# Attention stage of a fused attention and two-FFN kernel: order of one score product, one PSUM bank, SyncE's queue and VectorE's low parts

## The chip, the cores and the metric

The kernel runs on one core of a Trainium2 chip. The metric is the device time of one execution in microseconds (us). The core has TensorE (PE in the profile; its weight loads are PEld), VectorE (DVE), ScalarE (ACT), GpSimd (POOL) and SyncE (SP), which here only issues DMAs. Each engine runs its own instruction list in order and waits on semaphores.

## The reference, cut to what matters

```python
scores = scale * np.matmul(q, k.transpose(0, 1, 3, 2))      # B, H, S, D = 4, 8, 576, 64
scores = np.where(causal, -1e9, scores); scores -= scores.max(-1, keepdims=True)
a = np.exp(scores); a /= a.sum(-1, keepdims=True) + 1e-09
local = np.matmul(a, v)
q_p = phi(q)                                                # elu(q) + 1
mem_out = (q_p @ M_prev) / ((q_p @ z_prev)[..., None] + 1e-6)
attn = g * mem_out + (1 - g) * local                        # g = sigmoid(beta) per head
x = _moe_ref(attn as [2304, 512], ...)                      # silu(x @ w_gate) * (x @ w_val) @ w_out
return _moe2_ref(x, ...)                                    # g(x @ w_in) @ w_out
```

## The kernel before, in words

The 32 heads are worked off as 16 pairs. The 576 rows of a head are one block of 64 rows and four blocks ("tiles") of 128. A pair has four steps, tile 4 first (576 columns wide), then 3, 2 and 1 (448, 320, 192), and the two 64-row blocks of its heads together form one small product, F (`scores_f`, L1413 to L1419), that writes 64 columns of PSUM bank 1. Scores of tile 4 lie in banks 0 and 1 for the first head and in banks 2 and 3 for the second; tile 3 lies in bank 0 (first head) and bank 1 (second head); tiles 2 and 1 in banks 2 and 3.

TensorE's list is a software pipeline of rounds (L1530 to L1557). Round p holds: the scores of tile 4 of pair p; the "turns" of pair p-1 (transposes of the exponentiated rows, `turn`, in nine groups in the order of `TURNS`, each group in the PSUM bank that `BANK` names, group (1, 0) with one more transpose of the reciprocal sums); F of pair p; the last turn group (1, 1); the scores of tiles 3, 2 and 1 of pair p; and the products with the values of pair p-1 (`values`). F and tile 3 wait until VectorE has taken the maxima of both heads of tile 4 (semaphore `maxed`, one count per head). A turn group waits until the last content of its bank is copied away (`copied_under`).

VectorE's round p (L1161 to L1197): the reciprocal of the sums of pair p-1 (`sums_inverse`), the two outputs of pair p-2 (`out_x`, which need the broadcast sums `rbc`), the copy of turn group (4, 1), the maxima of tile 4, the copy of group (2, 1), `norm_q` and the maxima of tile 3, then `rnorm_q` (whose first instruction is L1064), the maxima of tiles 2 and 1 and of F, small scales (`mem_scale`), `phi` of the next pair, in rounds 5, 6, 8 and 9 a low part of a weight (`up_low`, L1131) and in rounds 10 to 16 a low part of the first FFN's input (`x_low`, L1140), and last `mem_scale(j + 3)` (L1098). The first maxima and exponentials of a tile are taken head after head.

ScalarE's round: `exp_q` of the next pair, copies of turn groups, the row of the sums into `rrow` (L838), exponentials of tile 4, the copy of the last turn group, exponentials of tiles 3, 2, 1 and F (L821, L826), then a high part (`up_high`, `x_high`). GpSimd's round: in rounds 2 to 7 sums for the weights (`up_sums`), in 8 and 9 a low part, in 10 to 13 sums for the input (`x_sum`, L755), then `mem_rows` for each tile (it waits for `mem_scale`), `phi_z`, `v_scale` (L687) and `relu_q` (L669).

SyncE's queue in round p: `load_qk(p + 1)`, `load_nat(p + 2)`, `load_v(p)`, then `write_r(p - 1)`, which writes the row of sums to DRAM in two DMAs, and `read_r(p - 1)`, which reads it back broadcast into `rbc`. After the 16 rounds the two FFNs follow: three products for every float32 product, in 804 of the 973 us, with TensorE busy throughout. Their code is not touched.

Of the kernel before, what the change touches and what calls it, by code (L numbers as in the profile page):

```python
# [14 lines left out]
def attention_two_ffns(nc, qk_in, nat_in, vm_in, beta, w_up, w_down, out):  # L15
# [9 lines left out]
    SLOTS = NT - 1  # L25
# [25 lines left out]
    HIGH_AT = ((3, 0, 0), (4, 0, 1), (5, 0, 2), (6, 1, 0), (7, 1, 1), (8, 1, 2))  # L51
    X_SUMS_AT = ((10, 1), (11, 3), (12, 5), (13, 6))
    X_ORDER = (0, 2, 4, 1, 3, 5, 6)
    X_HIGH_AT = tuple((9 + n, X_ORDER[n]) for n in range(7))
# [9 lines left out]
    def at_least(eng, sem, value):  # L64

        if value > 0:
            eng.wait_ge(sem, value)

    ctx = ExitStack()
    with ctx:  # L70
# [296 lines left out]
        def tile_of(j):  # L367

            return j // SLOTS, SLOTS - j % SLOTS
# [14 lines left out]
        TURNS = ((4, 0), (4, 1), (3, 0), (4, 2), (3, 1), (2, 0), (1, 0), (2, 1), (1, 1))  # L384
# [2 lines left out]

        BANK = {(4, 0): 4, (4, 1): 5, (4, 2): 6, (3, 0): 7, (3, 1): 4, (2, 0): 5, (2, 1): 6, (1, 0): 7, (1, 1): 5}  # L390


        VALUES = (2, 1, 4, 3)
# [74 lines left out]
        SCORE_F = 960  # L468


        def ends_pair(j, g):

            return tile_of(j)[1] == 1 and g == 0

        def r_rows(j):

# [18 lines left out]
        def _(sp):  # L495

            def load_qk(p):

                at_least(sp, scored, SLOTS * (p - 1))
                at_least(sp, scoredf, p - 1)  # L500
                sp.dma_start(qk[:, p % 2], qk_in[p]).then_inc(ld_qk[p % 2], 16)

            def load_nat(p):

                at_least(sp, q_z, 2 * (p - 1))
                sp.dma_start(nat[:, p % 2].rearrange("p k d -> p (k d)"), nat_in[p]).then_inc(ld_nat[p % 2], 16)
# [7 lines left out]
            def write_r(p):  # L514

                sp.wait_ge(r_row, p + 1)
                sp.dma_start(rsums[p, :, D:].rearrange("h (i n) -> i h n", n=P), rrow[1:NBLK, p % 2]).then_inc(r_out, 16)
                sp.dma_start(rsums[p:p + 1, :, 0:D], rrow[0:1, p % 2].rearrange("o (h n) -> o h n", h=2)).then_inc(r_out, 16)


            def read_r(p):

                sp.wait_ge(r_out, 32 * (p + 1))
                at_least(sp, x_done, 2 * (p - 1))
                for h in range(2):
                    sp.dma_start(rbc[D * h:D * h + D, p % 2], rsums[p, h:h + 1].broadcast_to([D, S])).then_inc(r_in[p % 2], 16)
# [78 lines left out]
            for p in range(1, NPAIR):  # L605
                if 1 < p and p + 1 < NPAIR:
                    load_qk(p + 1)
                if p + 2 < NPAIR:
                    load_nat(p + 2)
                if p > 1:  # L610
                    load_v(p)
                write_r(p - 1)
                read_r(p - 1)
            write_r(NPAIR - 1)
            read_r(NPAIR - 1)

# [187 lines left out]
        def _(act):  # L804
# [25 lines left out]
            def copy_pt(p, i, g):  # L830

                j = step_of(p, i)
                if j >= PTS:
                    act.wait_ge(pv_done, values_count(j - PTS))
                act.wait_ge(turned, turned_count(j, g))
                if ends_pair(j, g):
                    at_least(act, r_out, 32 * (p - 1))
                    nc.scalar.activation(rrow[0:NBLK, p % 2], r_rows(j), ACT.Copy).then_inc(r_row, 1)  # L838
                dst, src = group_ends(j, g)
                nc.scalar.activation(dst, src, ACT.Copy).then_inc(pt_act, 1)  # L840
# [204 lines left out]
        def _(dve):  # L1045
# [117 lines left out]
            for p in range(NPAIR + 2):  # L1163
                j = SLOTS * p
                if 0 < p <= NPAIR:
                    sums_inverse(p - 1)
                if p > 1:
                    out_x(p - 2, 1)
                    out_x(p - 2, 0)
                if 0 < p <= NPAIR:  # L1170
                    copy_pt(p - 1, 4, 1)
                if 0 < p < NPAIR:
                    tile_max(j)
                if 0 < p <= NPAIR:
                    copy_pt(p - 1, 2, 1)
                if p < NPAIR:
                    norm_q(p)
                    if p > 0:
                        tile_max(j + 1)
                    else:  # L1180
                        dve.wait_ge(gt_set, 3)
                    rnorm_q(p)
                    tile_max(j + 2)
                    mem_scale(j)
                    mem_scale(j + 1)
                    tile_max(j + 3)
                    mem_scale(j + 2)
                if p + 1 < NPAIR:
                    phi(p + 1)
                for m, u, n in HIGH_AT:  # L1190
                    if m == p - 1 and n > 0:
                        up_low(u, n)
                for m, n in X_HIGH_AT:
                    if m == p - 1:
                        x_low(0, n)
                if p < NPAIR:
                    mem_scale(j + 3)  # L1197

# [178 lines left out]
        def _(pe):  # L1377
# [11 lines left out]
            def scores(j):  # L1389

                p, i = tile_of(j)
                w, s = width(i), p % 2
                if j == 0:
                    pe.wait_ge(ld_first, 16)
                else:
                    at_least(pe, ld_qk[s], 16 * (p // 2 + 1))
                if i == SLOTS:
                    at_least(pe, maxed, 2 * j)
                    at_least(pe, maxedf, p)
                else:  # L1400
                    at_least(pe, maxed, 2 * SLOTS * p + 2)
                for a0, a1 in ((0, min(w, 512)), (512, w)):
                    if a1 <= a0:
                        continue
                    for h in range(2):
                        rows = slice(D * h, D * h + D)
                        col = score_col(i, h)
                        mm = nc.tensor.matmul(psf[:, col + a0:col + a1], qk[rows, s, P + q0(i):P + q0(i) + P],  # L1408
                                              qk[rows, s, P + S + a0:P + S + a1], start=True, stop=True)
                mm.then_inc(scored, 1)  # L1410


            def scores_f(p):  # L1413

                s = p % 2
                at_least(pe, ld_qk[s], 16 * (p // 2 + 1))
                at_least(pe, maxed, 2 * SLOTS * p + 2)
                nc.tensor.matmul(psf[:, SCORE_F:SCORE_F + D], qk[:, s, 0:P], qk[:, s, P + S:P + S + D],  # L1418
                                 start=True, stop=True).then_inc(scoredf, 1)  # L1419

            def turn(p, i, g):

                j = step_of(p, i)
                at_least(pe, expd, 2 * (j + 1))
                at_least(pe, memd, j + 1)
                if i == 1:
                    at_least(pe, expdf, p + 1)
                if copied_under(j, g):
                    pe.wait_ge(*copied_under(j, g))
                if group_bank(j, g) == 7:  # L1430
                    at_least(pe, x_done, 2 * p - 1)
                if group_bank(j, g) == 6:
                    at_least(pe, x_done, 2 * p)
                a, b = GROUPS[i][g]
                for c in range(a, b):
                    col = chunk_col(i, c)
                    mm = nc.tensor.transpose(ps[:, group_bank(j, g), (c - a) * P:(c - a + 1) * P],  # L1437
                                             rown[:, j % ROWN, col:col + P], ident[:])
                if ends_pair(j, g):
                    pe.wait_ge(rdend, p + 1)  # L1440
                    mm = nc.tensor.transpose(r_rows(j), rden[:, p % 2], ident[:])
                mm.then_inc(turned, 1)
# [90 lines left out]
            for p in range(NPAIR + 1):  # L1533
                if p < NPAIR:
                    scores(SLOTS * p)
                if p > 0:
                    for i, g in TURNS[:2]:
                        turn(p - 1, i, g)
                    if p == NPAIR:
                        product(0, 0)  # L1540
                    for i, g in TURNS[2:-1]:
                        turn(p - 1, i, g)
                if p == 0:
                    idle_products(4)
                if p < NPAIR:
                    scores_f(p)
                if p > 0:
                    turn(p - 1, *TURNS[-1])
                if p == NPAIR:
                    product(0, 1)  # L1550
                if p < NPAIR:
                    for k in range(1, SLOTS):
                        scores(SLOTS * p + k)
                if p == 0:
                    idle_products(8)
                if p > 0:
                    for i in VALUES:  # L1557
                        values(p - 1, i)
# [73 lines left out]
```

## Time and profile before

| | |
|---|---|
| median of 3 runs | 975.17 us (974.75 to 975.19) |
| the profiled execution's own time | 974.91 us |
| its span | 973.0 us |
| TensorE busy | 963.2 us, 99% of the span |
| VectorE, ScalarE, GpSimd busy | 692.2, 459.1, 336.2 us |
| granted TensorE clock | full in all 40 slices |
| chain that ended last | TensorE 92%, VectorE 3%, DMA 2%, ScalarE 1% |

The profile's span runs from the first to the last instruction of one execution. A busy TensorE is not proof of back-to-back work: short waits can hide between two modelled ends of pipelined matmuls, so the starts of instructions are read, not only the busy time. GpSimd's spans are rough. A round of TensorE is read from the start of the 512-wide scores of tile 4 to the next such start: 5.80 (round 0), 14.42, 24.68, 35.27, 45.59, 55.92, 66.25, 76.57, 86.90, 97.38, 107.71 (round 10), 118.17, 129.12, 140.06, 151.01 and 161.88 us (round 15); round 15 ends at 172.21 us.

### The profile page before, as it was taken

The numbers are of one execution on the slowest core, as the hardware profiler recorded it, in microseconds if no ns is written. First come the engines' busy times: TensorE is split into PE (matmuls) and PEld (weight loads), VectorE is DVE, ScalarE is ACT, GpSimd is POOL, SyncE is SP. The second block draws the span as 40 slices with busy tenths as digits, with TensorE's granted clock in tenths as the row PEclk, the third lists the DMA queues.
The fourth block names the chain that finished last, engine by engine and source line by source line (L and its number), as shares of the span: only waits on it lengthen the run. The fifth ranks groups of instructions, "written<-read, shape, count | busy, mean of one in ns | idle before, by whom it ended". The sixth has DMA issues, their size and how long they took to land.

```text
span 973.0 us, 19123 instructions
## 1 busy us (share of the span) xinstructions
PE 963.2 (99%) x6372; PEld 927.0 (95%) x6372; DVE 692.2 (71%) x1369; ACT 459.1 (47%) x940; POOL 336.2 (35%) x385
## 2 busy tenths in 40 slices
PE   8999999999999999999999999999999999999998
PEld 7778777999999999999999999999999999999998
DVE  6788999476667555557555569888887677867766
ACT  7899888654444222234222246545543334433331
POOL 5777775287781000100000157798410010000000
PEclk9999999999999999999999999999999999999999
DMA  6554543698778655555555544767775754538421
GB/s 243 175 170 154 165 149 102 233 339 291 285 246 314 238 200 216 222 218 213 218 196 195 198 147 169 249 239 284 273 270 222 256 197 162 228 129 302 144 101 66
DMA packets 46158, 204.74 MB, mean 210 GB/s; under 512 B 5488, under 2 KB 5872, under 8 KB 46064
## 3 DMA queue, kind: packets, MB, share of 16 engines
q1 hardware_dynamic: 45920, 203.52, 57.5%
q8 instruction: 55, 0.90, 0.4%
q14 instruction: 39, 0.32, 0.1%
q10 hardware_dynamic: 144, 0.00, 0.0%
HBM read 147.33 MB, written 56.17 MB: 209 GB/s over the span
## 4 chain that ended last, share of the span: by engine, by line
PE 92%; DVE 3%; DMA 2%; issue 1%; ACT 1%; POOL 0%; SPq 0%; DVEq 0%; ACTq 0%; POOLq 0%
PE ps L1467 27%; PE ps L1469 26%; PE ps L1468 26%; PE ps L1437 5%; PE ps L1408 4%; PE ps L1461 4%; DVE negs L1079 1%; DMA wu_r<-w_up 1%; DMA qk<-qk_in 1%; PE ps L1418 0%; ACT rown L821 0%; DVE norms L1064 0%; DMA rbc<-rsums 0%; DVE xt_l L1140 0%; DMA rsums<-rrow 0%
## 5 line engine op out<-in xcount | busy, mean ns | idle before, releaser
L1467 PE MATMUL ps<-xt_h,wu_h 128*128 128x384 f32 x840 | 281.5, 335 | 0.7 <-DVE wu_l L1131 0.5
L1469 PE MATMUL ps<-xt_h,wu_l 128*128 128x384 f32 x840 | 280.7, 334 | 0.0
L1468 PE MATMUL ps<-xt_l,wu_h 128*128 128x384 f32 x840 | 280.7, 334 | 0.0
L1467 PE MATMUL ps<-hid_h,wd_h 128*128 128x384 f32 x672 | 225.0, 335 | 0.7 <-issue 0.6
L1469 PE MATMUL ps<-hid_h,wd_l 128*128 128x384 f32 x672 | 224.5, 334 | 0.0
L1468 PE MATMUL ps<-hid_l,wd_h 128*128 128x384 f32 x672 | 224.5, 334 | 0.0
L1258 DVE TENSOR_TENSOR xy<-xy,ps 128x384 f32<-128x384 f32 x288 | 158.2, 550 | 70.1 <-PE ps L1469 69.7
L935 ACT ACTIVATE hid_h<-hid_r 128x768 fp32r<-128x768 f32 x84 | 70.8, 843 | 205.0 <-DVE hid_r L1232 140.3
L1467 PEld LDWEIGHTS ps<-xt_h,wu_h 128*128 128x128 f32 x840 | 157.7, 188 | 2.8 <-issue 0.8
L1468 PEld LDWEIGHTS ps<-xt_l,wu_h 128*128 128x128 f32 x840 | 157.7, 188 | 0.0
L1469 PEld LDWEIGHTS ps<-xt_h,wu_l 128*128 128x128 f32 x840 | 157.7, 188 | 0.0
L1467 PEld LDWEIGHTS ps<-hid_h,wd_h 128*128 128x128 f32 x672 | 126.1, 188 | 2.1 <-issue 1.9
L1468 PEld LDWEIGHTS ps<-hid_l,wd_h 128*128 128x128 f32 x672 | 126.2, 188 | 0.0
L1469 PEld LDWEIGHTS ps<-hid_h,wd_l 128*128 128x128 f32 x672 | 126.1, 188 | 0.0
L1236 DVE TENSOR_TENSOR hid_l<-hid_r,hid_h 128x768 fp32r<-128x768 f32 x84 | 86.7, 1032 | 37.2 <-ACT hid_h L935 37.1
L755 POOL TENSOR_TENSOR traw<-xy 128x384 f32<-128x384 f32 x20 | 23.1, 1179 | 239.3 <-PE ps L1469 239.3
L821 ACT ACTIVATE rown<-negs,nmax 128x576 f32<-128x576 f32 (+3 forms) x128 | 77.0, 602 | 5.7 <-DVE nmax L1079 4.6
L920 ACT ACTIVATE u2s<-ps 128x384 f32<-128x384 f32 x60 | 29.4, 490 | 100.0 <-PE ps L1469 100.0
L720 POOL TENSOR_TENSOR wu_l<-wu_r,wu_h 128x256 fp32r<-128x256 f32 x65 | 55.1, 877 | 58.2 <-ACT wu_h L850 58.1
L1213 DVE TENSOR_TENSOR hb<-u2s,ps 128x384 f32<-128x384 f32 x60 | 33.1, 551 | 52.2 <-PE ps L1469 52.2
L1079 DVE CUSTOM_DVE_ANT_0 negs<-ps,mask 128x576 f32<-128x576 f32 (+3 forms) x128 | 65.8, 551 | 4.7 <-PE ps L1408 4.7
L1242 DVE SCALAR_TENSOR_TENSOR tmp<-tmp 128x768 f32<-128x768 f32 x48 | 52.0, 1083 | 23.8 <-ACT tmp L950 23.5
(87 smaller groups left out, 1291.3 us busy)
## 6 DMA issues: line engine op xcount, KB each, us to landing
wu_l<-kept_ul SPq DMA_DIRECT2D x40, 896.0 KB, 7.5
wu_h<-kept_uh SPq DMA_DIRECT2D x40, 896.0 KB, 5.5
kept_uh<-wu_h SPq DMA_DIRECT2D x20, 896.0 KB, 6.4
kept_ul<-wu_l SPq DMA_DIRECT2D x20, 896.0 KB, 7.5
wd_h<-kept_dh SPq DMA_DIRECT2D x28, 512.0 KB, 3.8
wd_l<-kept_dl SPq DMA_DIRECT2D x28, 512.0 KB, 5.5
wu_r<-w_up SPq DMA_DIRECT2D x20, 512.0 KB, 5.3
qk<-qk_in SPq DMA_DIRECT2D x15, 640.0 KB, 4.9
```

The costliest lines, as they stand in the source:

```text
L720: low = nc.gpsimd.tensor_tensor(wu_l[u % 3][:, k], wu_r[u % 3][:, k], wu_h[u % 2][:, k - 1].bitcast(F32), ALU.subtract)
L821: nc.scalar.activation(head_rows(j)[:, h + (i == 1), D:D + w], negs[:, t % NEGS, 0:w], ACT.Exp, bias=nmax[:, p % 2, k:k + 1], scale=-1.0, ...
L935: nc.scalar.activation(hid_h[:, t % 6], hid_r[:, t % 6], ACT.Copy).then_inc(hh_done, 1)
L1079: nc.vector.tensor_tensor_reduce(negs[:, t % NEGS, 0:w], psf[:, col:col + w], mask[:, S - w:S], -(float(D) ** -0.5), 3.0e38, ALU.add, ALU. ...
L1236: nc.vector.tensor_tensor(hid_l[:, t % 6], hid_r[:, t % 6], hid_h[:, t % 6].bitcast(F32), ALU.subtract).then_inc(hl_done, 1)
L1242: nc.vector.scalar_tensor_tensor(tmp[:, r], tmp[:, r], 1.0, tmp[:, r], ALU.min, ALU.mult).then_inc(s_done, 1)
L1258: nc.vector.tensor_tensor(y, y, o, ALU.add).then_inc(evac, 1)
L1408: mm = nc.tensor.matmul(psf[:, col + a0:col + a1], qk[rows, s, P + q0(i):P + q0(i) + P], qk[rows, s, P + S + a0:P + S + a1], start=True, s ...
L1437: mm = nc.tensor.transpose(ps[:, group_bank(j, g), (c - a) * P:(c - a + 1) * P], rown[:, j % ROWN, col:col + P], ident[:])
L1467: nc.tensor.matmul(dst, w_hi, v_hi, start=start, stop=False, skip_group_check=onto)
L1468: nc.tensor.matmul(dst, w_hi, v_lo, start=False, stop=False, skip_group_check=onto)
L1469: return nc.tensor.matmul(dst, w_lo, v_hi, start=False, stop=stop, skip_group_check=onto)
```

## The change

The last turn group moves from bank 5 to bank 4. The reciprocal sums' transpose goes with group (2, 0) instead of (1, 0). On SyncE, `write_r(p - 1)` comes ahead of `load_nat(p + 2)` and `read_r(p - 1)` ahead of `load_v(p)`. VectorE's low parts move from behind `phi` to behind the maxima of tile 4. F and tile 3 wait for the maximum of tile 4's first head alone. The last turn group comes ahead of F.

```diff
-        BANK = {..., (2, 0): 5, (2, 1): 6, (1, 0): 7, (1, 1): 5}
+        BANK = {..., (2, 0): 5, (2, 1): 6, (1, 0): 7, (1, 1): 4}
-        def ends_pair(j, g):
-            return tile_of(j)[1] == 1 and g == 0
+        def with_sums(j, g):
+            return (tile_of(j)[1], g) == (2, 0)
@@ SyncE
+                write_r(p - 1)
                 if p + 2 < NPAIR:
                     load_nat(p + 2)
+                read_r(p - 1)
                 if p > 1:
                     load_v(p)
-                write_r(p - 1)
-                read_r(p - 1)
@@ ScalarE, copy_pt, and TensorE, turn
-                if ends_pair(j, g):
+                if with_sums(j, g):
@@ VectorE
                     tile_max(j)
+                for m, u, n in HIGH_AT:
+                    if m == p - 1 and n > 0:
+                        up_low(u, n)
+                for m, n in X_HIGH_AT:
+                    if m == p - 1:
+                        x_low(0, n)
                 if 0 < p <= NPAIR:
                     copy_pt(p - 1, 2, 1)
...
                     phi(p + 1)
-                for m, u, n in HIGH_AT:
-                    if m == p - 1 and n > 0:
-                        up_low(u, n)
-                for m, n in X_HIGH_AT:
-                    if m == p - 1:
-                        x_low(0, n)
                 if p < NPAIR:
                     mem_scale(j + 3)
@@ TensorE, scores
-                    at_least(pe, maxed, 2 * SLOTS * p + 2)
+                    at_least(pe, maxed, 2 * SLOTS * p + (1 if i == 3 else 2))
@@ TensorE, scores_f
-                at_least(pe, maxed, 2 * SLOTS * p + 2)
+                at_least(pe, maxed, 2 * SLOTS * p + 1)
@@ TensorE, the rounds
+                if p > 0:
+                    turn(p - 1, *TURNS[-1])
                 if p == 0:
                     idle_products(4)
                 if p < NPAIR:
                     scores_f(p)
-                if p > 0:
-                    turn(p - 1, *TURNS[-1])
```

## Rows read from the trace of the kernel before

**Rows 1.** Windows over whole rounds: label, us, busy us per engine, clock, DMA

```profile
35.27:107.71 72.44, 72.44 (x787) 58.41 (x785) 61.72 (x228) 65.36 (x194) 55.66 (x72) 1.00 0.50 164
107.71:118.17 10.46, 10.44 (x114) 8.41 (x113) 9.70 (x33) 9.40 (x29) 8.37 (x10) 1.00 0.43 144
118.17:151.01 32.84, 31.46 (x336) 25.39 (x337) 30.38 (x100) 28.84 (x85) 25.07 (x30) 1.00 0.49 155
151.01:161.88 10.87, 10.42 (x113) 8.44 (x113) 10.03 (x36) 10.23 (x33) 6.92 (x9) 1.00 0.43 134
```

**Rows 2.** Timeline, TensorE in round 5: start, us, operation, idle before and its releaser

```profile
60.08 0.49 PE L1437 MATMUL ps<-ident,rown 128*128 128x128 f32 x3
60.53 0.41 PE L1418 MATMUL ps<-qk 128*128 128x64 f32 x2
...
61.11 1.89 PE L1408 MATMUL ps<-qk 64*128 64x448 f32 x12
```

**Rows 3.** Timeline, TensorE in round 11

```profile
120.94 2.09 PE L1437 MATMUL ps<-ident,rown 128*128 128x128 f32 x16 [0.45 <-DVE xy L1125]
...
122.98 0.49 PE L1437 MATMUL ps<-ident,rown 128*128 128x128 f32 x3
123.31 0.33 PE L1418 MATMUL ps<-qk 128*128 128x64 f32 x2
```

**Rows 4.** Timeline, VectorE in round 5

```profile
56.38 0.16 DVE L1098 SCALAR_TENSOR_TENSOR mscale<-rsum,rnorm 128x3 f32<-128x3 f32 x1 [0.40 <-ACT rown L826]
...
59.63 0.75 DVE L1079 CUSTOM_DVE_ANT_0 negs<-ps,mask 128x576 f32<-128x576 f32 x1
...
60.68 0.56 DVE L1117 COPY pt<-ps 128x384 f32<-128x384 f32 x1 [0.29 <-PE ps L1437]
61.16 0.74 DVE L1059 TENSOR_REDUCE norm<-qz 128x9 f32<-128x576 f32 x1
62.18 0.62 DVE L1079 CUSTOM_DVE_ANT_0 negs<-ps,mask 128x448 f32<-128x448 f32 x1 [0.28 <-PE ps L1408]
```

**Rows 5.** Timeline, VectorE at the end of its round 11

```profile
126.06 1.01 DVE L1064 SCALAR_TENSOR_TENSOR norms<-norm,gt 128x9 f32<-128x9 f32 x1
...
129.84 1.15 DVE L1140 TENSOR_TENSOR xt_l<-xy,xt_h 128x768 fp32r<-128x768 f32 x1
```

**Rows 6.** Timeline, GpSimd in round 11

```profile
123.45 1.66 POOL L669 TENSOR_SCALAR qrelu<-nat 128x576 f32<-128x576 f32 x1
125.07 1.98 POOL L755 TENSOR_TENSOR xt_r<-xy,xt_r 128x384 f32<-128x384 f32 x2
```

**Rows 7.** Timeline, ScalarE in rounds 5 and 11

```profile
62.90 0.67 ACT L821 ACTIVATE rown<-negs,nmax 128x448 f32<-128x448 f32 x1
...
66.43 0.19 ACT L826 ACTIVATION_READ_ACCUMULATOR rown<-negf,nmax 128x1 f32 x1
...
127.82 0.56 ACT L821 ACTIVATE rown<-negs,nmax 128x320 f32<-128x320 f32 x1 [0.71 <-DVE nmax L1079]
```

**Rows 8.** Timeline, GpSimd in round 0

```profile
11.27 1.65 POOL L669 TENSOR_SCALAR qrelu<-nat 128x576 f32<-128x576 f32 x1
```

**Rows 9.** Timeline, VectorE in rounds 0 and 2

```profile
12.20 0.17 DVE L1064 SCALAR_TENSOR_TENSOR norms<-norm,gt 128x9 f32<-128x9 f32 x1
...
26.54 0.82 DVE L1125 TENSOR_TENSOR xy<-ps,rbc 128x320 f32<-128x320 f32 x2 [0.87 <-DMA rbc<-rsums]
```

**Rows 10.** Timeline, SyncE's queue in round 5: issue start, us, DMA

```profile
59.11 0.43 SPq L511 DMA_DIRECT2D vm<-vm_in  x1
60.65 0.68 SPq L517 DMA_DIRECT2D rsums<-rrow  x1
...
63.34 1.13 SPq L526 DMA_DIRECT2D rbc<-rsums  x2
```

**Rows 11.** Answer on one tile's rows (vm) and timeline, GpSimd in round 5

```profile
DMA to landing us min/median/max: 3.0/3.6/8.1
...
58.66 1.26 POOL L687 TENSOR_TENSOR vm<-vm,cf 128x640 f32<-128x640 f32 x1
```

More of the change, by code:

```diff
@@ L386, in attention_two_ffns @@
         ON_DVE = ((4, 1), (2, 1))
-        BANK = {(4, 0): 4, (4, 1): 5, (4, 2): 6, (3, 0): 7, (3, 1): 4, (2, 0): 5, (2, 1): 6, (1, 0): 7, (1, 1): 5}
+        BANK = {(4, 0): 4, (4, 1): 5, (4, 2): 6, (3, 0): 7, (3, 1): 4, (2, 0): 5, (2, 1): 6, (1, 0): 7, (1, 1): 4}
         VALUES = (2, 1, 4, 3)
@@ L1438, in turn @@
                                              rown[:, j % ROWN, col:col + P], ident[:])
-                if ends_pair(j, g):
+                if with_sums(j, g):
                     pe.wait_ge(rdend, p + 1)
```

## The prediction, made before the run

> **What bounds the kernel now.** The page comes first: TensorE is busy 99% of the span, 92% of the chain that ended last, and the clock is full in every slice. Only the attention stage, up to 172.21 us, is touched, so it is read round by round, with R for the start of a round and R' for the next. The view of windows shows two kinds. Rounds 3 to 9 take 72.44 us, 10.35 each, with TensorE never idle; rounds 11 to 13 take 32.84, 10.95 each, with TensorE idle 1.38 in all, and round 14 takes 10.87 [rows 1]. The two kinds have different limits.
>
> In round 5 (R = 55.92) TensorE's timeline has a wait that no idle column tells. Three transposes start at 60.08 and F at 60.53, 0.45 later; in round 11 the same step takes 0.33 [rows 2, 3]. The 0.12 between is F's wait for the second head of tile 4, whose maximum starts at 59.63 and takes 0.75 [rows 4]. This wait is there in rounds 1, 3 to 9 and 15, with 0.08 in round 10.
>
> In round 11 the limit is VectorE. TensorE stands 0.45 before bank 7's turns, for `out_x` [rows 3]; ahead of that on VectorE is a low part of 1.15, and further ahead L1064, which takes 1.01 where it takes 0.17 elsewhere [rows 5, 9]. It ends at 127.07, as GpSimd's `x_sum` does (125.07 + 1.98) [rows 6]: VectorE waits for GpSimd's instruction.
>
> **TensorE's own edits.** (1) The last turn group ahead of F, and one head instead of two: the first head's maximum is there from 59.71, long before F's place, and group (3, 1), which bank 4 now needs copied, is copied before (2, 0) on ScalarE. The transposes, F and tile 3 are the same instructions. From the first of the three transposes to tile 3 it was 61.11 - 60.08 = 1.03 [rows 2]; without the wait it is 0.91. I take 0.12 in each round bound by TensorE, so 10.21 a round. Bounds: 0 if the wait only moves, 0.25 if a switch from transposes to products goes too. Tile 2 still waits for both heads, whose end at 60.39 is before its turn. Rounds 1 and 3 to 9: 8 x 0.12 = 0.96. (2) The sums' transpose with group (2, 0): the same count of transposes, needing the reciprocal early in the round; 0 on TensorE. ScalarE copies the row some 0.4 earlier.
>
> **SyncE's edits.** The row's writes start at 60.65 now, 1.5 after `load_v` at 59.11, and the read back at 63.34 [rows 10]. They would start near 60.25 with no load's bytes ahead of them. In return `load_nat` (from 58.73 to some 61.6) is ahead of the read back and `load_v` is behind it, near 64.1 instead of 59.11. With the median landing of 3.6 [rows 11] v is there at 67.7; its user `v_scale` starts 58.66 + 10.33 = 69.0 [rows 11], a margin of 1.3. The q loads come 0.1 to 0.5 later, each with a round to spare. For the read back, landing at about 66.5 to 67, `out_x` starts near 67.2 and bank 7's turn can use it until 1.0 later; this cover would take a delay of 1 us. So 0 in most rounds, a gain in round 2: there `out_x` stands 0.87 for `rbc` [rows 9] and the round takes 10.59 instead of 10.33. With the row's write ahead of a load that is one part gone from the queue; the round falls to 10.21, a gain of 0.38 (bounds: -0.5, if the load ahead of the read back costs more than it frees, and 0.38). Rounds 1 to 9 together: 1.34.
>
> **The low parts.** They now start when the maxima of tile 4 end, at R + 4.47, and delay what follows: copy of (2, 1), `norm_q` and the maxima of tile 3. VectorE has idle time there, 0.29 and 0.28 [rows 4], so the maxima of tile 3 start at R + 6.6 instead of R + 6.26 with an input's part (0.98 alone), R + 6.4 with a weight's. The copy ends at R + 6.0, before `values` reads it at R + 6.9. What the delay reaches: ScalarE's exponentials of tile 3, which start at R + 6.98 and end with F's sum 3.72 later [rows 7], move by 0.3 to 0.45; then `mem_scale(j + 3)` and `out_x`. In place of that the low part is gone from behind `phi`.
> Call m the start of the last `mem_scale` after R: 0.46 in round 5 [rows 4]. GpSimd follows it: `v_scale` at m + 2.28 [rows 4, 11], `relu_q` 1.23 later, the end of `x_sum` 3.6 after that [rows 6], m + 7.11. L1064 ends at the later of that and R + 7.85. Round 12's start is 2.05 after L1064's end (129.12 - 127.07), and F's exponential ends 3.15 after it (0.75 to tile 2's [rows 7], then 3.72 less 1.32 for tile 3), so the next m is L1064's end + 3.24 less the round. Step by step: round 10 enters with m near 0.93, ends L1064 at 8.05, round 10.21; then m 1.08, 8.19, 10.25; m 1.18, 8.30, 10.36; and 10.36 again, the length of this loop through GpSimd. `out_x` is ready for bank 7 at m + 0.98 = 2.16, within what TensorE's turns leave (120.94 - 0.6 = R + 2.17). Round 14, without `x_sum`, and 15: 10.21 each.
> Rounds 10 to 15 were 10.46 + 32.84 + 10.87 + 10.33 = 64.50; they become 10.21 + 30.97 + 10.21 + 10.21 = 61.60: a gain of 2.90 (bounds below: -6, the lock rival; above 3.24 with all six at 10.21). Rounds 5, 6, 8 and 9 stay at 10.21: m rises to 0.7, under a cover of 0.7.
>
> **What this rests on** is that a low part, which reads two tensors in SBUF, runs beside `relu_q`, which fills R + 3.97 to R + 5.6. Against GpSimd's TENSOR_TENSOR L1064 waits to its end [rows 5, 6]. Against `relu_q`, a TENSOR_SCALAR, one row speaks: in round 0 it runs from 11.27 to 12.92 [rows 8] and L1064 starts at 12.20 and takes 0.17 [rows 9]. Same instruction, same size, not held. It is one row, of a tiny operation.
> The Trainium skill, page "SBUF — State Buffer", section "Who interferes with whom", says that a VectorE instruction with two SBUF inputs contends with any GpSimd instruction that reads SBUF, and that whichever came first keeps the shared ports for its whole length. By that `relu_q` would hold the low part back; the trace agrees for TENSOR_TENSOR (1.01 against 0.17) and disagrees for TENSOR_SCALAR. The first rival below is what the rule would do here.
>
> **The sum.** 1.34 + 2.90 = 4.24 us. The profiled execution took 974.91 (span 973.0 and 1.9 around it), which gives 970.7; it is 0.26 under the median of the runs, 975.17, which gives 970.9. The tail after 172.21 moves as a whole: its last low part moves ahead into 2.32 us in which VectorE stands, its reads have no loads around them. I predict 971.0. Within 0.2%, 1.95 us, is what a measurement can't tell from no change.
>
> **Rivals.** (a) *`relu_q` holds the low parts.* Then one starts at m + 5.12 instead of R + 4.47, right when GpSimd's next instruction would. Round 5: start 5.58, L1064's end 5.58 + 0.75 + 2.41 = 8.74, round 10.79, next m 1.19; from a round that enters so: start 6.31, 9.47, round 11.52. With an input's part (0.98): 9.70, 11.75. Rounds 5, 6, 8, 9: 44.6 against 41.5, +3.1; rounds 10 to 15: 70.5 against 64.5, +6.0; the other five give back 0.9. Total +8.2: 983.3, slower. It decides as soon as the hold is over some 0.5. For it: [rows 5, 6], the same two engines one operation further. Against it: [rows 8, 9]. (b) *The low part holds `relu_q`*, which then runs 0.98 longer; `x_sum` ends that much later, the loop through GpSimd is 11.3: rounds 10 to 13 +1.7 in all, round 9 +0.6, rounds 14 and 15 -0.8, the rest -1.2: about 975.5, no change. For it: GpSimd's small products beside `phi` take 0.82 for 0.4. Against: `relu_q` took its usual 1.65 beside L1064. (c) *Late loads*: v lands after `v_scale`'s turn. Its longest landing was 8.1 [rows 11]; a delay of 1 us in each of the four `x_sum` rounds goes straight into them, +4: 975. Against: the margin of 1.3. (d) *The wait of F only moves*, to tile 3 or the last turn's bank: 1 us less gain, 972.
>
> **How the numbers follow.** Forecast with (d) inside: 0.63, own range 970.0 to 972.8. (a) 0.18, (b) 0.09, (c) 0.05, mixtures of small gains and losses 0.05. Faster by over 0.2%: 0.65, the forecast and part of the mixtures; within: 0.15, mainly (b) and (c); slower: 0.20. The range from 969.8 to 976.5 takes in the forecast, (b) and (c), and leaves out (a) and little else.
>
> **What would show it.** Right: F 0.25 before tile 3's switch and 1.03 down to 0.91; rounds 5, 6, 8, 9 at 10.21; low parts at R + 4.47 with 0.75 to 1.0 each beside `relu_q` of 1.65; no idle before bank 7; L1064 still over 0.17 in rounds 11 to 13; no wait for `rbc` in round 2. Wrong: low parts of 1.8 or more, rounds of 11 and over (a); `relu_q` of 2.6 (b); idle before L687 for vm (c); an idle of TensorE before L1418 or the last L1437 (d).

## The result and the profile after

The changed kernel takes 970.33 us in the median of 7 runs (969.60 to 972.71), the kernel before 975.17: ratio 0.9955 over all runs (the two medians alone give 0.9950), 95% interval 0.9945 to 0.9964. Predicted were 971.0 and 969.8 to 976.5.

The profiled execution took 969.61 us, with a span of 967.7 (before 974.91 and 973.0). Windows over whole rounds (label, us, busy us of TensorE, its weight loads, VectorE, ScalarE, GpSimd, clock, DMA share, GB/s), the changed kernel:

```profile
34.75:74.80 40.05, 40.05 (x451) 33.38 (x449) 34.83 (x131) 36.49 (x109) 30.90 (x40) 1.00 0.52 168
74.80:85.57 10.77, 10.20 (x115) 8.35 (x113) 9.03 (x33) 9.94 (x32) 8.23 (x11) 1.00 0.45 155
85.57:95.58 10.01, 10.01 (x114) 8.34 (x112) 8.93 (x34) 9.01 (x28) 8.10 (x11) 1.00 0.50 170
95.58:106.23 10.65, 10.20 (x115) 8.34 (x113) 9.55 (x34) 9.60 (x31) 8.57 (x12) 1.00 0.49 164
106.23:116.45 10.22, 10.21 (x114) 8.35 (x113) 9.39 (x33) 9.17 (x28) 8.30 (x10) 1.00 0.57 164
116.45:147.24 30.79, 30.52 (x338) 25.14 (x337) 28.61 (x100) 28.81 (x85) 26.52 (x30) 1.00 0.52 168
147.24:157.47 10.23, 10.23 (x112) 8.44 (x112) 9.67 (x35) 9.88 (x31) 7.19 (x9) 1.00 0.36 124
```

Set them beside [rows 1]. Rounds 3 to 6 take 10.01 each (10.33 before), rounds 11 to 13 30.79 (32.84), round 14 10.23 (10.87). Rounds 7 and 9 stand out with 10.77 and 10.65, TensorE idle 0.57 and 0.45 in them: `out_x` on VectorE waits for the broadcast sums `rbc`, and TensorE for `out_x`. In round 7:

```profile
77.05 0.82 DVE L1125 TENSOR_TENSOR xy<-ps,rbc 128x320 f32<-128x320 f32 x2 [0.63 <-DMA rbc<-rsums]
...
77.69 1.61 PE L1437 MATMUL ps<-ident,rown 128*128 128x128 f32 x13 [0.57 <-DVE xy L1125]
```

Rounds 1 to 9 went from 93.29 to 91.56 us, rounds 10 to 15 from 64.50 to 61.27, the rest after round 15 from 800.8 (the 804 given for the two FFNs in the description of the kernel is found in no row) to 800.2; round 1 starts 0.25 later.

TensorE in round 5 (R = 54.77), from the timeline (start, us, operation, idle before and its releaser):

```profile
56.00 2.56 PE L1437 MATMUL ps<-ident,rown 128*128 128x128 f32 x21
58.40 0.27 PE L1441 MATMUL ps<-ident,rden 128*9 128x128 f32 x1
58.51 1.04 PE L1437 MATMUL ps<-ident,rown 128*128 128x128 f32 x8
59.38 0.33 PE L1418 MATMUL ps<-qk 128*128 128x64 f32 x2
59.65 1.89 PE L1408 MATMUL ps<-qk 64*128 64x448 f32 x12
```

Eight transposes from 58.51 to 59.38 are 0.109 each, so the last five are 0.54, and with F's 0.27 it is 0.82 where [rows 2] have 1.03: F's 0.12 of wait is gone, and another 0.09, which I put down to the transposes no longer being interrupted by F.

The low parts beside `relu_q`, VectorE and GpSimd of the changed kernel:

```profile
58.82 1.64 POOL L669 TENSOR_SCALAR qrelu<-nat 128x576 f32<-128x576 f32 x1
59.16 0.87 DVE L1131 TENSOR_TENSOR wu_l<-wu_r,wu_h 128x512 fp32r<-128x512 f32 x1
...
69.11 1.64 POOL L669 TENSOR_SCALAR qrelu<-nat 128x576 f32<-128x576 f32 x1
69.17 1.14 DVE L1131 TENSOR_TENSOR wu_l<-wu_r,wu_h 128x512 fp32r<-128x512 f32 x1
...
110.61 1.50 DVE L1140 TENSOR_TENSOR xt_l<-xy,xt_h 128x768 fp32r<-128x768 f32 x1
110.63 1.65 POOL L669 TENSOR_SCALAR qrelu<-nat 128x576 f32<-128x576 f32 x1
...
131.20 0.95 DVE L1140 TENSOR_TENSOR xt_l<-xy,xt_h 128x768 fp32r<-128x768 f32 x1
131.30 2.35 POOL L669 TENSOR_SCALAR qrelu<-nat 128x576 f32<-128x576 f32 x1
133.63 1.97 POOL L755 TENSOR_TENSOR xt_r<-xy 128x384 f32<-128x384 f32 x2
134.28 0.37 DVE L1064 SCALAR_TENSOR_TENSOR norms<-norm,gt 128x9 f32<-128x9 f32 x1
```

A 768-wide low part that meets nothing takes 0.95. From it I estimate 0.68 for 512: VectorE's copies of 512 elements take 0.69 in this profile and those of 384 take 0.54 to 0.56, so 256 elements less are about 0.27 less. Then the first three pairs have one reading: the low part gets going 0.53 us after `relu_q` started (59.16 + 0.87 - 0.68 = 59.35; 69.17 + 1.14 - 0.68 = 69.63; 110.61 + 1.50 - 0.95 = 111.16), whenever it came; the low parts at 89.95, 100.40 and 141.41, which take 0.88, 0.94 and 1.48 beside `relu_q` at 89.61, 100.13 and 141.42, give 0.54, 0.53 and 0.52. `relu_q` holds it for the first third of its 1.65 and no longer. Where the low part is first by 0.1, `relu_q` takes 2.35 instead. One rival is that the hold is a tail of `v_scale`, a TENSOR_TENSOR that ends where `relu_q` starts. Rows of the round where a low part starts during `v_scale` speak against it:

```profile
119.96 1.25 POOL L687 TENSOR_TENSOR vm<-vm,cf 128x640 f32<-128x640 f32 x1
120.84 1.19 DVE L1140 TENSOR_TENSOR xt_l<-xy,xt_h 128x768 fp32r<-128x768 f32 x1
```

Here the low part gets going at 120.84 + 1.19 - 0.95 = 121.08, 0.13 before `v_scale` ends, and `relu_q` waits in its turn.

In round 12 L1064 now comes during the first of `x_sum`'s two instructions and waits 0.2 for its end, where [rows 5] show it just behind the start of the second one, waiting 0.84.

### The profile page after: what moved, and what is told of

Its sections match the earlier page's. It is cut to its first block, busy times and chain, and to the rows that moved or that the text cites. A ratio compares the mean times of both kernels' runs of the same rounds, so it can differ in the third digit from the quotient of the medians.

```text
span 967.7 us, 19123 instructions
## 1 busy us (share of the span) xinstructions
PE 959.4 (99%) x6372; PEld 927.0 (96%) x6372; DVE 691.0 (71%) x1369; ACT 458.5 (47%) x940; POOL 338.1 (35%) x385
## 4 chain that ended last, share of the span: by engine, by line
PE 95%; DVE 2%; DMA 1%; POOL 1%; issue 1%; ACT 1%; SPq 0%; ACTq 0%; DVEq 0%; POOLq 0%
PE ps L1467 27%; PE ps L1469 26%; PE ps L1468 26%; PE ps L1437 5%; PE ps L1461 5%; PE ps L1408 4%; DMA rbc<-rsums 1%; DVE xt_l L1140 1%; PE ps L1384 0%; DMA rsums<-rrow 0%; PE ps L1418 0%; DVE negs L1079 0%; DVE hid_r L1232 0%; POOL wd_l L729 0%; PE ps L1441 0%
## 5 line engine op out<-in xcount | busy, mean ns | idle before, releaser
L950 ACT ACTIVATE tmp<-hb,nhalf 128x768 f32<-128x768 f32 x48 | 45.1, 940 | 46.5 <-DVE hb L1213 34.5
```

The source lines that it names most:

```text
L950: nc.scalar.activation(tmp[:, r], hb[:, u % 2, r], ACT.Relu, bias=nhalf[:], scale=0.5).then_inc(relued, 1)
```

## The experiments

In what follows, full clock means a mean granted clock of 1.000 over the execution. Eight kernels take the change apart or put one piece back (e), four build on it (g); each has a median, and a count of the executions whose mean granted clock was 0.998 and not 1.000 (all runs of the kernel before beside them were at 1.000).

| kernel | us (runs) | of these at 0.998 |
|---|---|---|
| changed kernel | 970.33 (7) | 5 |
| e1 TensorE's edits alone | 970.73 (5) | 4 |
| e2 one head alone | 974.38 (11) | 6 |
| e3 SyncE's order alone | 975.69 (11) | 0 |
| e4 low parts alone | 972.67 (8) | 0 |
| e5 changed, sums with (1, 0) | 973.48 (11) | 6 |
| e6 changed, read back ahead of load_nat | 976.65 (12) | 6 |
| e7 changed, relu_q with two inputs | 973.34 (10) | 4 |
| e8 changed, low parts back | 970.57 (5) | 1 |
| g1 changed, 13 idle products | 968.73 (5) | 0 |
| g2 as g1, SyncE's order of before | 969.09 (5) | 0 |
| g3 as g1, order nat, writes, read back, v | 967.98 (5) | 0 |
| g4 as g3, low parts back | 968.18 (5) | 0 |

Before: 975.12 beside e1 to e4, 974.97 beside e5 to e8, 974.82 beside g1 to g3, 974.68 beside g4.

**e1, TensorE's edits alone.** The kernel before with these hunks of the change:

```diff
-        BANK = {..., (1, 0): 7, (1, 1): 5}
+        BANK = {..., (1, 0): 7, (1, 1): 4}
-            return tile_of(j)[1] == 1 and g == 0
+            return (tile_of(j)[1], g) == (2, 0)
-                    at_least(pe, maxed, 2 * SLOTS * p + 2)
+                    at_least(pe, maxed, 2 * SLOTS * p + (1 if i == 3 else 2))
-                at_least(pe, maxed, 2 * SLOTS * p + 2)
+                at_least(pe, maxed, 2 * SLOTS * p + 1)
+                if p > 0:
+                    turn(p - 1, *TURNS[-1])
...
-                if p > 0:
-                    turn(p - 1, *TURNS[-1])
```

> The kernel before with TensorE's edits alone (last turn group in bank 4 and ahead of F, sums with group (2, 0), one head's maximum for F and tile 3). Theory 1, every TensorE-bound round loses 0.32 us (10.33 to 10.01: 0.12 of F's wait, 0.10 of one switch between transposes and products less, 0.10 of the stall before group (1, 0) filled by the sums' transpose): rounds 1, 3 to 9 and 15 give 2.6 to 2.9 us, rounds 11 to 14 stay at 10.9, time 972.4, ratio 0.9972. Theory 2, only F's 0.12 comes from TensorE and the other 0.20 of the changed kernel's rounds is a gift of the moved low parts or of the queue: 9 x 0.12 = 1.1 us, 974.1, ratio 0.9989.

Ratio 0.9955 (0.9943 to 0.9968), the whole gain of the change. Rounds 2 to 9 are 10.01 to 10.24, as theory 1 says. But it fails on rounds 11 to 14: they take 10.67, 11.02, 10.01 and 10.01, not 10.9, with the low parts still behind `phi`. VectorE and GpSimd in round 13 of e1:

```profile
144.62 1.98 POOL L755 TENSOR_TENSOR xt_r<-xy,xt_r 128x384 f32<-128x384 f32 x2
145.41 0.25 DVE L1064 SCALAR_TENSOR_TENSOR norms<-norm,gt 128x9 f32<-128x9 f32 x1
148.45 1.16 DVE L1140 TENSOR_TENSOR xt_l<-xt_r,xt_h 128x768 fp32r<-128x768 f32 x1
```

L1064 starts 0.79 after `x_sum` and slips in between its two instructions; in the kernel before it starts 0.99 after it [rows 5, 6]. In round 10 of e1 it still takes 0.96, and round 11 is long (10.67) because `out_x` is late behind it; round 12 (11.02) is long by a wait of 0.88 for `rbc`. That TensorE's scores of tile 3, which come earlier, are what shifts L1064 is my reading; no run moves them alone.

**e2, one head alone.**

```diff
-                    at_least(pe, maxed, 2 * SLOTS * p + 2)
+                    at_least(pe, maxed, 2 * SLOTS * p + (1 if i == 3 else 2))
-                at_least(pe, maxed, 2 * SLOTS * p + 2)
+                at_least(pe, maxed, 2 * SLOTS * p + 1)
```

> The kernel before, only F and tile 3 wait for one head instead of two; order and banks stay. Theory 1: 0.12 us in each of 9 rounds, steady rounds 10.21, time 974.1. Rival: behind F's wait the last turn group, still in bank 5, waits for the copy of (2, 0), which ends at R + 4.5, so the 0.12 only moves there: 975.2, steady rounds 10.33.

974.38; eight rounds at 10.22 or 10.23, so the 0.12 (here 0.11) is real and does not move to bank 5. TensorE in round 5 of e2:

```profile
60.90 0.49 PE L1437 MATMUL ps<-ident,rown 128*128 128x128 f32 x3
61.22 0.33 PE L1418 MATMUL ps<-qk 128*128 128x64 f32 x2
61.48 0.41 PE L1437 MATMUL ps<-ident,rown 128*128 128x128 f32 x2
61.81 1.89 PE L1408 MATMUL ps<-qk 64*128 64x448 f32 x12
```

From the first transpose to tile 3 it is 0.91, as the prediction has it. The last two transposes, between F and tile 3, take 0.33 here and 0.22 in the changed kernel, ahead of F: there the further 0.09 lies.

The five executions at full clock have a median of 973.2, the six others 974.6: the same edit brings the drop of the clock described below.

**e3, SyncE's order alone.** The kernel before with this hunk:

```diff
+                write_r(p - 1)
                 if p + 2 < NPAIR:
                     load_nat(p + 2)
+                read_r(p - 1)
                 if p > 1:
                     load_v(p)
-                write_r(p - 1)
-                read_r(p - 1)
```

> The kernel before with SyncE's new order alone (writes of the sums, load_nat, read back, load_v). Theory 1: only round 2 gains, 0.3 us, as the row's write has no load ahead: 974.9. Rival: the load now ahead of the read back makes rbc late in some rounds, as in rounds 7 and 9 of the changed kernel (10.77 and 10.65): with slower rounds (10.33) the cover is 0.3 greater, but up to 1 us is lost: 976.

Ratio 1.0006 (0.9997 to 1.0015). Round 2 falls from 10.59 to 10.33, as said, and round 3 takes 10.70 in its place, with a wait for `rbc` of 0.9. So no gain, and perhaps 0.6 us of loss that the interval does not separate from none.

**e4, low parts alone.** The kernel before with these lines moved from behind `phi` into the middle of the round:

```diff
+                for m, u, n in HIGH_AT:
+                    if m == p - 1 and n > 0:
+                        up_low(u, n)
+                for m, n in X_HIGH_AT:
+                    if m == p - 1:
+                        x_low(0, n)
```

> The kernel before with the low parts moved behind tile 4's maxima, nothing else. Theory 1 (the multiply-free TENSOR_SCALAR relu_q holds the shared access only for its first 0.53 us): rounds 11 to 14 fall from 10.95 to about 10.4, round 10 and 15 stay near 10.35, time 972.8; low parts take 0.68 (512) or 0.95 (768) plus what is left of the 0.53. Rival (relu_q holds it throughout): low parts of 1.8 and more, rounds of 11 and over, 983.

Ratio 0.9976 (0.9966 to 0.9986), rounds 10 to 14 at 10.36, 10.33, 11.06, 10.37, 10.33; the 11.06 has a wait of 0.98 for `rbc`. The 768-wide low parts take 0.95 to 1.45: theory 1. In round 10 of e4:

```profile
112.24 1.65 POOL L669 TENSOR_SCALAR qrelu<-nat 128x576 f32<-128x576 f32 x1
112.27 1.45 DVE L1140 TENSOR_TENSOR xt_l<-xy,xt_h 128x768 fp32r<-128x768 f32 x1
```

Alone the move is worth 2.5 us, and 2.5 + 4.4 of e1 less 0.6 of e3 is 6.3, against 4.8 for all three together.

**e5, the sums' transpose back at group (1, 0).**

```diff
-            return (tile_of(j)[1], g) == (2, 0)
+            return tile_of(j)[1] == 1 and g == 0
```

> The changed kernel with the sums' transpose back at group (1, 0). Theory 1: group (1, 0) then stands about 0.1 us for the copy of (3, 0) out of bank 7, steady rounds 10.11 instead of 10.01, and the row is written 0.45 later, so the cover of the read back shrinks: 971.5 to 972.5. Rival: the place of the sums' transpose is free on TensorE: rounds 10.01, 970.4.

973.48, worse than expected; the five executions at full clock have 972.35, inside the range of theory 1, and the six others 973.9. The undisturbed rounds are 10.11, so 0.10 is the place of the sums' transpose. My reason for it, that at (2, 0) it fills a stall of TensorE before (1, 0), is argued: no row shows this stall. Much of the rest is `rbc`: nine waits of VectorE, 4.6 us in all, of which 1.1 reach TensorE in the profile, for a row whose write starts 4.85 behind the round's start (51.93 in round 4) in place of 4.37 (59.14 in round 5 of the changed kernel).

**e6, read back ahead of load_nat.**

```diff
                 write_r(p - 1)
+                read_r(p - 1)
                 if p + 2 < NPAIR:
                     load_nat(p + 2)
-                read_r(p - 1)
```

> The changed kernel with the read back ahead of load_nat too (write, read back, load_nat, load_v). Theory 1: the waits for rbc in rounds 7 and 9 (0.57 and 0.45 us of TensorE) come from load_nat's bytes ahead of the read back; they go, 969.3, and the runs scatter less. Rival: they come from something else on the queue (spread of the landings), and the wait of SyncE for the write's landing now also delays both loads by 1: 970.3 or, if v then comes late, 971 and over.

Ratio 1.0020 (1.0011 to 1.0029). Theory 1 fails. The rival has the direction (971 and over), but it looked to v, whose waits are the smaller part. Waits of e6 from 30 to 170 us (engine, what it waited for, us in total, times, longest):

```profile
ACT qexp L810 <- DMA nat<-nat_in: 10.4, 11, 1.6
...
PE ps L1437 <- ACT pt L840: 5.4, 9, 1.6
...
POOL vm L687 <- DMA vm<-vm_in: 2.2, 4, 0.8
```

The waits for `rbc` are gone, but `load_nat` now stands behind SyncE's wait for the writes' landing, and `exp_q` of the next pair, which heads ScalarE's round, waits for it: ScalarE's copies of the turn groups come late, and TensorE waits for a bank. The issue of that load in the changed kernel and in e6, each in its round 5 (which starts at 54.77 and at 55.19):

```profile
60.53 0.39 SPq L506 DMA_DIRECT2D nat<-nat_in  x1
```

```profile
63.09 0.58 SPq L506 DMA_DIRECT2D nat<-nat_in  x1
```

It is issued 7.90 behind the round's start in place of 5.76.

**e7, relu_q as an instruction with two inputs.** It adds zero to q in place of the relu, which is left out.

```diff
-                nc.gpsimd.tensor_scalar(qrelu[:], nat[:, p % 2, 0:NBLK], 0.0, None, ALU.max)...
+                nc.gpsimd.tensor_tensor(qrelu[:], nat[:, p % 2, 0:NBLK], zero, ALU.add)...
```

> The changed kernel with relu_q as a two-input TENSOR_TENSOR (q + 0 in place of max(q, 0): the relu is left out). If it is GpSimd's kind of instruction that decides how long VectorE's two-input instructions are held: low parts are held to its end, 1.8 us and more, rounds 5, 6, 8, 9 at 10.6 to 11.3, rounds 10 to 15 near 11.3 to 11.6, time 978 to 983. Rival (the hold depends on something else, such as the place in the round): low parts as now, 0.87 to 1.5, and 970.3.

973.34, 3.0 over the changed kernel (972.9 in the six executions at full clock). Rows of e7 (one line is added ahead, so L670 is `relu_q`, L1132 and L1141 the low parts):

```profile
61.10 1.40 POOL L670 TENSOR_TENSOR qrelu<-nat,mask 128x576 f32<-128x576 f32 x1
61.44 1.60 DVE L1132 TENSOR_TENSOR wu_l<-wu_r,wu_h 128x512 fp32r<-128x512 f32 x1
...
123.43 1.40 POOL L670 TENSOR_TENSOR qrelu<-nat,mask 128x576 f32<-128x576 f32 x1
123.63 2.02 DVE L1141 TENSOR_TENSOR xt_l<-xy,xt_h 128x768 fp32r<-128x768 f32 x1
```

By the same reckoning the low part gets going at 61.44 + 1.60 - 0.68 = 62.36 and 123.63 + 2.02 - 0.95 = 124.70, 1.26 and 1.27 after `relu_q`'s start: all but its last 0.13. The kind of GpSimd's instruction decides, as expected; the price was overrated (978 to 983), since `relu_q` is shorter in this form (1.40) and in five of nine rounds the low part comes first, takes 0.92 to 1.21 and makes GpSimd wait.

**e8, low parts back behind phi**, the rest as in the changed kernel:

```diff
-                for m, u, n in HIGH_AT:
-                    if m == p - 1 and n > 0:
-                        up_low(u, n)
-                for m, n in X_HIGH_AT:
-                    if m == p - 1:
-                        x_low(0, n)
...
```

> The changed kernel with the low parts back behind phi. Theory 1: rounds 11 to 14 go back to 10.95, their limit is the loop through GpSimd, not TensorE; rounds 5, 6, 8, 9 stay at 10.01: 970.3 + 3 = 973.3. Rival: with TensorE's round shorter by 0.32 the low parts of rounds 5, 6, 8, 9 also come onto the path: 974.5.

970.57, where both theories wanted 973 and more. The four executions at full clock have 970.2. In its profile L1064 takes 1.01 in round 10 and 0.70 in round 12, and rounds 11 and 13 behind them are 10.67 and 10.44; rounds 12 and 14, with 10.52 and 11.61, have waits for `rbc` of 0.38 and 1.48. So the stall of L1064 is not quite gone here, but it no longer comes in every round.

**The clock.** Executions at 0.998 have one round 1 of 11.6 instead of 10.0. In the profile of e1, TensorE's timeline and then windows of 1 us (clock is the third number from the end):

```profile
14.38 1.85 PE L1408 MATMUL ps<-qk 64*128 64x512 f32 x8 [2.09 <-DVE nmax L1085]
16.16 3.58 PE L1437 MATMUL ps<-ident,rown 128*128 128x128 f32 x21
```

```profile
15.00:16.00 1.00, 1.00 (x8) 0.56 (x4) 0.54 (x4) 1.00 (x5) 0.59 (x2) 0.50 1.01 412
16.00:17.00 1.00, 1.00 (x7) 0.88 (x6) 0.05 (x1) 0.00 (x0) 1.00 (x3) 0.50 1.01 414
17.00:18.00 1.00, 1.00 (x7) 1.00 (x6) 0.00 (x0) 0.60 (x1) 1.00 (x2) 0.50 1.01 414
```

From 15 to 18 us the granted clock is 0.50, the 1.2 GHz level, and 21 transposes take 3.4 us instead of 2.35. Ahead of it TensorE stood idle for 2.09 us. The same row in the kernel before, in the changed kernel (whose profiled execution is one at full clock) and in g1:

```profile
14.42 1.30 PE L1408 MATMUL ps<-qk 64*128 64x512 f32 x8 [1.38 <-DVE nmax L1085]
```

```profile
14.67 1.30 PE L1408 MATMUL ps<-qk 64*128 64x512 f32 x8 [1.97 <-DVE nmax L1085]
```

```profile
14.37 1.30 PE L1408 MATMUL ps<-qk 64*128 64x512 f32 x8 [0.98 <-DVE nmax L1085]
```

The one-head wait lets TensorE run through round 0 some 0.6 us earlier (the row of F starts at 8.84 in the kernel before, behind 0.65 idle, and at 8.10 in e1), into a wait for F's maximum that ends no sooner.

**g1, 13 idle products** in place of 8 at the end of round 0.

```diff
-                    idle_products(8)
+                    idle_products(13)
```

> The changed kernel with 13 instead of 8 idle products at the end of round 0 (1.3 us more of TensorE's idle time filled, nothing else). Theory 1: the one-head wait lets TensorE run through round 0 early and stand 2.0 us before round 1 instead of 1.38; in the executions whose mean clock is 0.998 the granted clock is 1.2 GHz in part of round 1, which takes 11.6 instead of 10.0. With the idle time down to 0.7 all executions stay at 1.000: median 969.6, down from 970.33, highest under 971. Rival: the drop has another cause (the weight of the stretch before): the share of 0.998 executions stays 5 in 7 and the median 970.3.

968.73 (968.09 to 970.35), TensorE idle 0.98 there, all five executions at 1.000. Theory 1. The edit both shortens the idle time and gives TensorE more work before it; which of the two keeps the clock up is not separated. The median is also 0.9 under the two executions of the changed kernel at full clock (969.60 and 969.61), so not all of the 1.6 is the clock; five runs and two do not tell where the rest comes from.

**g2 and g3, SyncE's order**, on top of g1: in g2 nat, v, writes, read back, as before the change; in g3:

```diff
-                write_r(p - 1)
                 if p + 2 < NPAIR:
                     load_nat(p + 2)
+                write_r(p - 1)
                 read_r(p - 1)
```

> As the kernel with more idle products, and SyncE's order as before (nat, v, writes, read back). Theory 1: the new queue order costs what it did alone (975.69 against 975.12, +0.6), in waits for rbc in single rounds like 7 and 9 of the changed kernel: 968.9 to 969.3. Rival: with rounds of 10.01 the loads ahead of the writes come too close to the read back and rbc is late more often: 970.3 and a wider spread.

> As the kernel with more idle products, with SyncE's order nat, writes, read back, v: no load's bytes between the writes and the read back, nat early for exp_q, v behind. Theory 1: the waits for rbc go, since load_nat stands 1.5 us ahead of the writes and is nearly landed: 968.6. Rival: load_nat ahead delays the writes' landing as much as it delayed the read back: 969.6.

g2 969.09, g3 967.98 (967.60 to 968.63), its ratio to before 0.9931 (0.9918 to 0.9943). g3 lies under g1 and g2 in the median and has the narrowest spread, with two waits for `rbc`, of 0.9 in all. Five runs each do not separate the three by their intervals. The 969.09 lies in theory 1's range for g2, but g2 is not faster than g1, which that theory needs; so neither theory of g2 is shown.

**g4, low parts back** on top of g3, by the edit of e8.

> The fastest so far (13 idle products, SyncE's order nat, writes, read back, v; 967.98) with the low parts back behind phi. Theory 1 (TensorE's edits alone already carry L1064 past GpSimd's second x_sum instruction, so the low parts' move is worth little): rounds 10 to 14 between 10.0 and 10.7, time 968.0 to 969.2. Rival (the two gains add, as predicted): rounds 11 to 14 back at 10.9 with L1064 at 1.0, time 971.

968.18, ratio 0.9930 (0.9916 to 0.9944), no difference from g3. L1064 in its rounds 10 and 11:

```profile
112.25 0.97 DVE L1064 SCALAR_TENSOR_TENSOR norms<-norm,gt 128x9 f32<-128x9 f32 x1
...
123.05 0.17 DVE L1064 SCALAR_TENSOR_TENSOR norms<-norm,gt 128x9 f32<-128x9 f32 x1
```

It pays its whole price once, in round 10, which makes round 11 take 10.76 (g3 10.23); in rounds 11 to 13 it takes 0.17 to 0.25, and rounds 12 to 14 are 10.01, 10.02 and 10.00, where g3, with the low parts in the middle, has 10.12, 10.12 and 10.16. The two come to the same. The rival, that the two gains add, is refuted. g3 and g4 are faster than both kernels of the case; g3 is 2.3 us faster than the changed one.

## Why the prediction was right, and where not

The total held: 4.24 us were forecast, 4.84 measured in the medians and 5.3 between the profiled executions. The terms held less well, and their errors partly cancelled, which is luck. TensorE's edits gave 0.32 a round and not 0.12, and waits for `rbc` in rounds 7 and 9 (0.76 and 0.64 over 10.01) took 1.4 of it back: rounds 1 to 9 give 1.73 where 1.34 was forecast. And the median of 970.33, near the 971.0, is of an execution with a stretch of low clock that the prediction does not know; at full clock it is 969.6.

- **TensorE's own edits**, step (1), 0.12 a round: mis-sized. Together with the sums' transpose it is 0.32. The 0.12 is shown by e2 (10.22), 0.09 more by the transposes in one piece (the rows of round 5 of e2 and of the changed kernel), which the step named within its upper bound of 0.25 and did not take, and step (2), "0 on TensorE", is 0.10, shown by e5.
- **SyncE's edits**: "this cover would take a delay of 1 us" failed. The read back landed in 2.8 to 4.9 us (2.8 to 4.2 before), and rounds 7 and 9 stand 0.57 and 0.45 for `out_x`. The gain of round 2 came (10.11, and 10.33 in e3), and was spent elsewhere. Rival (c), late v, did not come: one wait of 0.2.
- **The low parts**: -2.90 forecast for rounds 10 to 15, -3.23 measured, and e4 gives 972.67 where 972.8 was expected of it, with the loop of the prediction. But the step treated this gain as one that adds to TensorE's. It does not: e1 has most of it without the move (rounds 10 to 14 in 51.75, the changed kernel 51.24, before 54.17), and g4 all of it (50.84, with the move in g3 50.72). Before the change L1064 arrived just as `x_sum`'s second instruction started, each round anew, and paid its whole length; arriving 0.1 to 0.2 sooner, from the round after on, is as good as moving the low part. Either of the two edits would have removed the stall; the changed kernel has both and is paid for one.
- **What this rests on**: the one row of round 0 was read rightly, but it starts 0.93 after `relu_q` does and so could not show a hold of 0.53; that the hold is no longer than this was luck. Rival (a), that `relu_q` holds the low parts throughout, is refuted by the rows above and e4; that it holds them for 0.53 was missed, and costs at most 0.55. Rival (b), that the low part holds `relu_q`, is half true: `relu_q` took 2.35 in three rounds, without the price, as L1064 then waits 0.2 and not 0.8. The Trainium skill's rule (page "SBUF — State Buffer", section "Who interferes with whom") has it right that the two instructions contend and that the first one goes first; its "for the whole instruction" holds here for GpSimd's TENSOR_TENSOR (e7: all but 0.13 of 1.40) and not for its TENSOR_SCALAR (0.53 of 1.65).
- **Not in the prediction at all**: round 0 and the clock. I costed the one-head wait in rounds 1 to 15 and not in round 0, where it lengthens an idle time from 1.38 to some 2.0 us. Five of the seven executions show the drop, and their median is 0.9 us above that of the two others (970.48 against 969.60), where the one long round of a profile costs 1.6; in g1 no execution shows it.

## What to carry to other kernels

Two engines that alternate on a shared resource can settle into a phase. Here a stall that came back in every round, with the length of one whole instruction of the other engine, went by either of two edits that shifted one engine a little; the gains of several such edits must not be added. When a wait is relaxed, look also at the first round, where the engine may only reach a longer idle time sooner, and read the granted clock behind it. Before a DMA is moved behind another's landing, list every user of what it brings: here v had 1.3 us to spare by the estimate of the prediction and waited once, for 0.2, and nat, whose user heads the next round of another engine, did not have the 2.1 us by which e6 issues its load later.

## What the runs showed of the hardware that was not expected

GpSimd's TENSOR_SCALAR of 576 elements delays VectorE's instruction with two inputs in SBUF only until 0.53 us after its start (six pairs, 0.52 to 0.55), its TENSOR_TENSOR of the same size until 1.26 us of 1.40. In e1, behind 2.09 us of standing idle, TensorE's granted clock fell to 1.2 GHz 0.6 us after work had begun again and stayed there for some 3 us. The profiles of e2, e5, e7 and e8 show the same drop behind 2.11, 2.05, 2.30 and 2.04 us; those of the changed kernel and of e6, with 1.97 and 1.99, do not. A mean clock of 0.998, which goes with such a stretch, was found in 32 of the 61 executions of the seven kernels whose profiles have a gap of 1.97 to 2.30 us there, and in none of the others, with 1.37 or 1.38 us or 0.8 to 1.0.
